# Answers in the banks of the scores with crossed heads, and a down product in a bank of its own in two halves

## The chip, the cores and the metric

The kernel runs on one core of one Trainium2 chip. The metric is the device time of one execution in microseconds (us). Five engines work in parallel, each through its own instruction stream and in order: PE (TensorE, matmuls and transposes), DVE (VectorE), ACT (ScalarE), POOL (GpSimd) and SP (SyncE, which issues most DMAs here). They are tied by semaphores. PE writes to PSUM, which has eight banks of 512 float32 columns by 128 partitions.

## What is computed

```python
# 4 batches, 8 heads, 768 steps, 48 channels a head
for t in range(S):                       # complex decay a, real input k v^T, real answer q S_re
    new_re = ar * S_re - ai * S_im
    new_im = ar * S_im + ai * S_re
    S_re, S_im = new_re + kv, new_im     # kv = k_t v_t^T per head, 48 x 48
    y[:, :, t] = einsum('bhd,bhde->bhe', q[:, :, t], S_re)
x = y laid out as (3072 tokens, 384)
x = max(x @ w1, x @ w2, x @ w3) @ w_out  # 384 -> 768 -> 384
# then a mixture of 8 experts: argmax routing, relu(x @ w1[e]) @ w2[e], gate
```

`a` is scaled to a magnitude of at most 0.999 first.

## The kernel before

The 3072 tokens are 24 chunks of 128. The program has two parts. The first is a loop over n = 0 to 25, which I call stages, written out by hand for each engine: the order of the calls in the source is the order on the engine. The second (from about 622 us) is the expert part, which the change does not touch.

Stage n works on three chunks at once:

- Chunk n, attention. `scores(n)` (PE, L1758) makes k·q for 8 heads into `sc` (two banks, 512 columns each). DVE's `mask(n)` (L1176) turns them into `att`. `keys_back(n)` (PE, L1768) transposes the keys into `tr`, ACT's `kp_copy` takes them out, `outer(n)` (PE, L1779) makes k v^T into the second bank of `yu`, DVE's `add_state` (L1201) adds it to the state, `rotation` (L1186 to L1191) decays the state. `answers(n)` (PE) has two pieces: `att` times v (L1791), and the old state times q (L1799), both into the first bank of `yu`. These last ones I call the state products. In chunks 0, 6, 12 and 18 a batch begins, and they are left out. ACT's `y_copy` (L739, L740) moves the answers to `y_end` and `x_raw`, SP moves small pieces between these two (`move_x`), ACT's `moe_x_hi` (L752) and DVE's `moe_x_lo` (L1152) split the result into two float32r parts.
- Chunk n-1, up products. `moe_up(t, g)` for g = 0 to 5 (PE, L1701, L1702, L1705: nine matmuls of 384 columns) goes to the two banks of `mm` in turn. ACT's `moe_copy` takes groups 0 and 3 into `h_sb`; DVE's `moe_max` (L1164) takes the maximum with groups 1, 2, 4 and 5.
- Chunk n-2, down product. `moe_ht` (PE, L1732) transposes `h_sb` into `tr` in halves, ACT's `moe_h_hi` (L763) and DVE's `moe_h_lo` (L1169) split it, `moe_down` (18 matmuls of 392 columns) writes to the second bank of `mm`, and ACT's `moe_out` (L769, L772, L774) reads it three times. `moe_up` group 1 of chunk n-1 needs the same bank, and waits on `x2_taken` for that.

A transposed `h_sb` half needs both of its maxima: `moe_ht(t, half)` waits on `p_maxed` for 4t + 2 half + 2.

Beside this runs the decay of `a`. Two chunks make a group (g = 0 to 11). Its 16 steps in a row are multiplied up by POOL (`chain_steps`, L2069 to L2073), its four blocks are joined by DVE (`join`, L1144 to L1148), ACT lays the result out (`stage_z`), and DVE makes decayed q and k for chunk n+1 from it (`z_norm` L1207, `z_newton`, `q_decay`, `k_decay`, up to L1233). The raw `a` is scaled ahead of that by ACT and DVE (`norm_square` to `norm_apply`, L1087 to L1117), stored to a scratch in device memory by SP, and loaded again in the layout of the chain (`load_ring`). So POOL's group g waits on a DMA which waits on DVE's `norm_apply` in an earlier stage. Tables (`norms_in`, `joins_early`, `joins_late`) say in which stage each of these steps stands; from group 6 on a group has one join late in stage 2g-3, one early and one late in stage 2g-2.

On PE a stage stands as: scores of two head pairs, transpose of the first half of chunk n-2, scores of the other pairs, up group 0, transpose of the second half, the whole down product, keys back, up group 1, outer, up group 2, answers, up groups 3 to 5.

Of the kernel before, what the change touches and what calls it, by code (L numbers as in the profile page):

```python
# [41 lines left out]
def attention_moe_program(nc, first_d, a_d, q_d, k_d, v_d, w_up, w_dn, emb, tau, e1, e2, q, k, v, a_re, a_im, an_d, x2_dram, out):  # L42
# [23 lines left out]
    with ctx:  # L66
# [595 lines left out]
        def _(act):  # L662
# [73 lines left out]
            def y_copy(n):  # L736
                act.wait_ge(y_done, n + 1)
                wait(act, xt_ready, n)
                nc.scalar.activation(y_end[:, :], yu[0:R, 0, KX * P:FREE], ACT.Copy).then_inc(y_copied, 1)  # L739
                nc.scalar.activation(x_raw[0:R, :, :], yu[0:R, 0, 0:KX * P].rearrange("p (k t) -> p k t", t=P), ACT.Copy).then_inc(y_copied, 1)  # L740

            def moe_copy(t, half):
                act.wait_ge(p_done, 6 * t + 3 * half + 1)
                if half == 0:
                    wait(act, ht_done, 2 * t)
# [20 lines left out]
            def moe_out(t, tile=None):  # L766
                at = ds(t if tile is None else tile, 1)
                act.wait_ge(x2_done, t + 1)
                nc.scalar.activation(z_all[:, at, :].rearrange("p t e -> p (t e)"), mm[:, 1, HD:NX], ACT.Copy) \  # L769
                    .then_inc(x2_taken, 1)  # L770
                wait(act, x2_stored, 16 * t)
                nc.scalar.activation(x2_sb[:, :], mm[:, 1, 0:HD], ACT.Copy).then_inc(x2_ready, 1)  # L772
                wait(act, x2_taken, 2 * t)
                nc.scalar.activation(mm[:, 1, 0:HD], mm[:, 1, 0:HD], ACT.Square,  # L774
# [78 lines left out]
            for n in range(NC + 2):  # L853
# [11 lines left out]
                if prev2:  # L865
                    moe_h_hi(n - 2, 0)
# [32 lines left out]
                if n == 0:  # L899
                    low_copy(range(14, 16))  # L900
                for m in norms:
                    norm_rsqrt(m, norm_of(m))
                for m in later[:1]:
                    norm_square(m, norm_of(m))
                if now:
                    y_copy(n)
                if n == 0:
                    low_copy(range(16, LOWS - KF + 3))
                if prev:
                    moe_copy(n - 1, 1)  # L910
# [3 lines left out]
            def steps(b):  # L914
                with act.Fori(0, CB) as part:
# [7 lines left out]
                    for x, (bank, dst) in enumerate(((sc, col_re), (tr, col_im), (sc, col_q), (tr, col_k))):  # L923
# [6 lines left out]
                    nc.scalar.activation(y_rows[:, :, :, 0:D], yu[:, 0, 0:KX * 2 * D].rearrange("p (k b d) -> p k b d", k=KX, b=2), ACT.Copy) \  # L930
                        .then_inc(y_copied, 1)
                    for x in range(KX):
                        ins = nc.scalar.activation(y_rows[:, x, :, D:HALF],
                                                   yu[:, 0, KX * 2 * D:HD].rearrange("p (b k r) -> p k b r", k=KX, b=2)[:, x, :, :], ACT.Copy)
# [1315 lines left out]
```

## Time and profile before

| | |
|---|---|
| time, median of 3 runs | 939.7 us (937.9 to 940.3) |
| the profiled execution | 938.67 us |
| its span in the profile | 936.9 us |
| PE busy | 836.2 us (89%) |
| DVE busy | 661.6 us (71%) |
| ACT busy | 441.9 us (47%) |
| POOL busy | 518.3 us (55%) |

A time line has the start and the length in us, the engine, the line, the output and inputs, the shape, the count, and in brackets the idle time just before with what ended it. "Mean ns" is that of one instruction. A float32 matmul (not float32r) is two rows in the profile. Busy shares are averages over stages with different limits, so the table does not name the bound of any one stage.

### The profile page before, as it was taken

The page shows a single profiled execution, that of the slowest core. Times are in us where ns is not written, and L with a number is a line of the kernel's source. Part 1 is how long each engine was busy: PE and PEld are TensorE (multiplying, and loading weights), DVE is VectorE, ACT ScalarE, POOL GpSimd, SP SyncE. Part 2 cuts the span into 40 slices and gives each one's busy share as a digit, 9 for nine tenths or more (in the row PEclk, how much of TensorE's full clock was granted, in tenths as well). Part 3 has the DMA queues.
Part 4 walks back from the last instruction along what each step waited for, and adds up shares of the span by engine and source line. Part 5 has one row for each costly group of instructions (what it writes and reads, how often), then busy time and mean ns, then how long its engine had stood idle before and what let it go on. Part 6 is the DMA issues. An engine that isn't in the chain of part 4 may idle for free.

```text
span 936.9 us, 18639 instructions
## 1 busy us (share of the span) xinstructions
PE 836.2 (89%) x6641; PEld 765.7 (82%) x6642; DVE 661.6 (71%) x1066; ACT 441.9 (47%) x817; POOL 518.3 (55%) x886
## 2 busy tenths in 40 slices
PE   0568899998998999999999999958999999999995
PEld 0445788887977898888898899857999999998894
DVE  5989789998897999999977755357533262647731
ACT  5686646574654566565443443231321142436611
POOL 1199989799999999998894000002332332324222
PEclk9769799999999999999999999985999999999998
DMA  9401142451424242432311110333711124236311
GB/s 304 117 20 31 65 112 83 100 163 56 130 63 101 73 124 80 110 84 64 90 41 41 51 56 20 107 121 128 280 59 34 42 64 165 94 126 225 129 35 43
DMA packets 41874, 89.72 MB, mean 96 GB/s; under 512 B 6264, under 2 KB 23680, under 8 KB 40480
## 3 DMA queue, kind: packets, MB, share of 16 engines
q1 hardware_dynamic: 37632, 76.04, 26.6%
q0 software_dynamic: 4160, 12.60, 4.0%
q8 instruction: 50, 0.82, 0.4%
q14 instruction: 32, 0.26, 0.1%
HBM read 69.74 MB, written 17.69 MB: 93 GB/s over the span
## 4 chain that ended last, share of the span: by engine, by line
PE 53%; POOL 17%; DVE 15%; issue 6%; ACT 5%; DMA 2%; SPq 1%; ACTq 0%; DVEq 0%; POOLq 0%
PE mm L1701 6%; PE mm L1705 5%; PE mm L1702 5%; POOL c_im L2070 4%; PE yu L1701 4%; POOL c_re L2069 4%; PE yu L1705 4%; PE yu L1702 4%; POOL ring L2073 4%; POOL ring L2072 3%; PE sc L1758 2%; PE tr L1970 2%; PE mm L1972 2%; PE tr L1972 2%; PE mm L1970 2%
## 5 line engine op out<-in xcount | busy, mean ns | idle before, releaser
L1701 PE MATMUL mm<-up_hi,x_hi 128*128 128x384 f32 x432 | 156.8, 363 | 23.0 <-ACT mm L774 9.7
L1702 PE MATMUL mm<-up_lo,x_hi 128*128 128x384 f32 x432 | 147.1, 341 | 0.0
L2069 POOL TENSOR_TENSOR c_re<-ring 112x128 f32<-112x128 f32 x165 | 104.3, 632 | 59.9 <-DVE ring L1117 36.2
L2070 POOL TENSOR_TENSOR c_im<-ring 112x128 f32<-112x128 f32 x165 | 118.8, 720 | 0.0
L2149 POOL DMA_INDIRECT out_rows<-g_o,rows_out x30 | 36.0, 1200 | 147.0 <-DVE g_o L1553 139.6
L1701 PEld LDWEIGHTS mm<-up_hi,x_hi 128*128 128x128 f32 x432 | 81.6, 189 | 38.8 <-ACT mm L774 14.7
L1705 PE MATMUL mm<-up_hi,x_lo 128*128 128x384 f32 x432 | 100.3, 341 | 3.0 <-DVE x_lo L1152 3.0
L2073 POOL TENSOR_TENSOR ring<-c_re,c_im 112x64 f32<-112x64 f32 x165 | 101.1, 613 | 0.0
L2125 POOL DMA_INDIRECT g_in<-x_scratch,rows_in x34 | 37.6, 1106 | 101.5 <-DVE rows_in L1516 76.1
L2072 POOL TENSOR_TENSOR ring<-c_re,c_im 112x64 f32<-112x64 f32 x165 | 83.9, 509 | 12.9
L1164 DVE TENSOR_TENSOR h_sb<-mm,h_sb 128x384 f32<-128x384 f32 x96 | 52.9, 552 | 46.7 <-PE mm L1705 44.9
L1705 PEld LDWEIGHTS mm<-up_hi,x_lo 128*128 128x128 f32 x432 | 78.8, 192 | 4.6 <-DVE x_lo L1152 4.6
L1701 PE MATMUL yu<-e_hi,gh_hi 128*128 128x384 f32 x240 | 82.4, 343 | 0.0
L1702 PEld LDWEIGHTS mm<-up_lo,x_hi 128*128 128x128 f32 x432 | 82.0, 190 | 0.0
L1702 PE MATMUL yu<-e_lo,gh_hi 128*128 128x384 f32 x240 | 80.9, 337 | 0.0
L1553 DVE TENSOR_SCALAR g_o<-yu,table_gate 128x384 f32 (+1 forms) x30 | 18.5, 617 | 70.3 <-POOLq L2145 36.1
L996 ACT ACTIVATE gh_hi<-tr 128x512 fp32r<-128x512 f32 x24 | 14.3, 598 | 102.5 <-PE tr L1972 98.0
L1418 DVE TENSOR_TENSOR e_lo<-raw,e_hi (+2 forms) x40 | 56.2, 1433 | 6.6 <-ACT e_hi L957 6.5
L1758 PE MATMUL sc<-q_t,k_t 48*128 48x128 f32 x768 | 57.7, 293 | 1.4 <-issue 1.2
L1758 PEld LDWEIGHTS sc<-q_t,k_t 48*128 48x128 f32 x768 | 48.9, 195 | 12.2 <-issue 12.2
L1701 PE MATMUL mm<-dn_hi,h_hi 128*128 128x392 f32 x144 | 51.9, 360 | 0.1
L1702 PE MATMUL mm<-dn_lo,h_hi 128*128 128x392 f32 x144 | 49.3, 343 | 0.0
(263 smaller groups left out, 2251.7 us busy)
## 6 DMA issues: line engine op xcount, KB each, us to landing
raw<-in_moe_w SPq DMA_DIRECT2D x16, 1536.0 KB, 9.0
a_dn<-in_a_laid SPq DMA_DIRECT2D x18, 384.0 KB, 7.0
an_scratch<-a_dn SPq DMA_DIRECT2D x18, 384.0 KB, 2.3
ring<-an_scratch SPq DMA_DIRECT2D x18, 384.0 KB, 5.8
q_in<-in_q_laid SPq DMA_DIRECT2D x24, 224.0 KB, 3.0
k_in<-in_k_laid SPq DMA_DIRECT2D x24, 224.0 KB, 3.1
v_in<-in_v_laid SPq DMA_DIRECT2D x24, 192.0 KB, 3.3
x_scratch<-x_sb SPq DMA_DIRECT2D x24, 192.0 KB, 2.6
```

The lines of the kernel that those rows point to most:

```text
L1164: nc.vector.tensor_tensor(hh, mm[:, (3 * half + w) % 2, 0:FH], hh, ALU.max).then_inc(p_maxed, 1)
L1418: nc.vector.tensor_tensor(flat(lo), flat(raw), flat(hi).bitcast(F32), ALU.subtract).then_inc(expert_lo, 1)
L1701: nc.tensor.matmul(out, hi[:, x, :], w_hi(x), start=(x == 0), stop=False)
L1702: nc.tensor.matmul(out, hi[:, x, :], w_lo(x), start=False, stop=False)
L1705: last = nc.tensor.matmul(out, lo[:, x, :], w_hi(x), start=False, stop=(x == K - 1))
L1758: last = nc.tensor.matmul(sc[:, b, h * P:(h + 1) * P], k_t[rows, x, h, :], q_t[n % 2][rows, x, h, :], start=(x == 0), stop=(x == 1))
L1970: nc.tensor.matmul(out, w_hi, x_hi[:, x, :], start=(x == 0), stop=False)
L2069: nc.gpsimd.tensor_tensor(c_re[:, 0:count, :, :], cur, bc(prev[:, :, 0, :], 2, 2), ALU.mult).then_inc(chain_prod, 1)
L2070: nc.gpsimd.tensor_tensor(c_im[:, 0:count, :, :], cur, bc(prev[:, :, 1, :], 2, 2), ALU.mult).then_inc(chain_prod, 1)
L2072: nc.gpsimd.tensor_tensor(cur[:, :, 0, :], c_re[:, 0:count, 0, :], c_im[:, 0:count, 1, :], ALU.subtract).then_inc(chain_step, 1)
L2073: nc.gpsimd.tensor_tensor(cur[:, :, 1, :], c_re[:, 0:count, 1, :], c_im[:, 0:count, 0, :], ALU.add).then_inc(chain_step, 1)
L2125: pool.indirect_dma_start(g_in[:, x, :], None, x2_dram, bass.IndirectOffsetOnAxis(ap=rows_in[x][:, :].bitcast(U32), axis=0)) \
```

## The change

It moves three things and reorders the stages around them.

1. The answers go to the two banks of `sc` (`answer_at`: columns 128, 512, 896 and 384 of the 1024) once the mask has read the scores. In head pairs 1 and 2 the two heads change sides (`side_of`): the head in partitions 0 to 47 of q and the state gives its answer to partitions 64 to 111. The weights w1 to w3 are laid out to match on the host. The state products are issued for two head pairs together, so that four in a row use the four combinations of row half and column half of the array. `scores(n+1)` now waits on `y_copied` for chunk n.
2. The down product goes to the first bank of `yu`, in two calls of nine matmuls. Group 1 of the up product no longer waits on `x2_taken` but on `p_maxed` (4t).
3. The first half of `h_sb` is transposed at the end of stage n-1 instead of in stage n, and split there.

```diff
             def moe_up(t, groups):
-                free = ((p_maxed, 4 * t - 1), (x2_taken, 2 * t), (p_copied, 2 * t + 1),
+                free = ((p_maxed, 4 * t - 1), (p_maxed, 4 * t), (p_copied, 2 * t + 1),
...
+            def moe_down(t, half):
+                out = yu[:, 0, 0:NX]
+                part = range(half * KX, (half + 1) * KX)
+                if half == 0:
+                    wait(pe, x2_taken, 2 * t)
+                pe.wait_ge(hh_ready, 2 * t + half + 1)
+                for x in part:
+                    nc.tensor.matmul(out, h_hi[:, x, :], dn_hi[:, x, :], start=(x == 0), stop=False)
+                    nc.tensor.matmul(out, h_hi[:, x, :], dn_lo[:, x, :], start=False, stop=False)
+                pe.wait_ge(ht_ready, 2 * t + half + 1)
+                for x in part:
+                    last = nc.tensor.matmul(out, h_lo[:, x, :], dn_hi[:, x, :], start=False, stop=(x == KF - 1))
...
+                    for both in ((0, 1), (3, 2)):
                         for x in range(2):
-                            for b in range(2):
-                                rows = rows_of(b)
-                                last = nc.tensor.matmul(yu[rows, 0, h * P:(h + 1) * P], st_t[rows, x, h, :], q_t[n % 2][rows, x, h, :],
-                                                        start=False, stop=(x == 1 and h == HP - 1))
+                            for h in both:
+                                for b in range(2):
+                                    rows = rows_of(b)
+                                    last = nc.tensor.matmul(answer[rows_of(side_of(h, b)), answer_at(h):answer_at(h) + P], st_t[rows, x, h, :],
+                                                            q_t[n % 2][rows, x, h, :], start=False, stop=(x == 1 and h >= 2))
...
 # PE's loop
                 if now:
-                    scores(n, range(0, HP // 2))
-                if prev2:
-                    moe_ht(n - 2, 0)
-                if now:
-                    scores(n, range(HP // 2, HP))
+                    scores(n)
...
+                if prev2:
+                    moe_down(n - 2, 0)
+                    moe_ht(n - 2, 1)
...
                     moe_up(n - 1, range(0, 1))
                 if prev2:
-                    moe_ht(n - 2, 1)
-                    moe_down(n - 2)
+                    moe_down(n - 2, 1)
...
-                if prev:
+                if prev and late_z:
                     moe_up(n - 1, range(2, 3))
                 if now:
                     answers(n)
+                if prev and not late_z:
+                    moe_up(n - 1, range(2, 3))
                 if prev:
-                    moe_up(n - 1, range(3, 6))
+                    moe_up(n - 1, range(3, 5))
+                    moe_ht(n - 1, 0)
+                    moe_up(n - 1, range(5, 6))
```

`late_z` is true in stages 1, 3 and 5 only. Three places show what stands in a row on an engine.

PE at the head of stage 15, from the scores to the second half's transpose and the down product. First as it stood, then as it stands; `tr<-ident,h_sb` is a transpose of `h_sb`, `dn_` the down weights, `up_` the up weights.

```order
L1758 MATMUL sc<-q_t,k_t 128x128 [waits masked,k_decayed,q_decayed]
L1758 MATMUL sc<-q_t,k_t 128x128 x7
L1732 MATMUL tr<-ident,h_sb 128x128 [waits p_maxed]
L1732 MATMUL tr<-ident,h_sb 128x128 x2
L1758 MATMUL sc<-q_t,k_t 128x128 x8
L1701 MATMUL mm<-up_hi,x_hi 128x384 [waits xh_ready,p_maxed]
```

```order
L1780 MATMUL sc<-q_t,k_t 128x128 [waits y_copied,k_decayed,q_decayed]
L1780 MATMUL sc<-q_t,k_t 128x128 x15
L1764 MATMUL yu<-dn_hi,h_hi 128x392 [waits hh_ready,x2_taken]
L1765 MATMUL yu<-dn_lo,h_hi 128x392
L1764 MATMUL yu<-dn_hi,h_hi 128x392
L1765 MATMUL yu<-dn_lo,h_hi 128x392
L1764 MATMUL yu<-dn_hi,h_hi 128x392
L1765 MATMUL yu<-dn_lo,h_hi 128x392
L1768 MATMUL yu<-dn_hi,h_lo 128x392 [waits ht_ready]
L1768 MATMUL yu<-dn_hi,h_lo 128x392 x2
L1754 MATMUL tr<-ident,h_sb 128x128 [waits p_maxed]
L1754 MATMUL tr<-ident,h_sb 128x128 x2
```

Group 0 comes next. Half of the down product now stands ahead of it, and so does the transpose of the second half, which waits for the last maximum of chunk n-2.

DVE at the head of stage 15, from the first split to the first maximum of the stage, before and after; `h_sb<-mm,h_sb` is a maximum, `a_dn` the scaled `a`, `att` the mask.

```order
L1164 TENSOR_TENSOR h_sb<-mm,h_sb 128x384 [waits p_maxed,p_copied,p_done] x2
L1152 TENSOR_TENSOR x_lo<-x_raw,x_hi 128x384 [waits xh_ready]
L1169 TENSOR_TENSOR h_lo<-tr,h_hi 128x384 [waits hh_ready]
L1114 SCALAR_TENSOR_TENSOR n_m<-n_la,n_rr 128x384 [waits rest_ready]
L1117 TENSOR_TENSOR a_dn<-a_dn,n_m 128x768 [waits scale_ready]
L1087 SCALAR_TENSOR_TENSOR n_m<-n_sq 128x384 [waits a_normed,asq_ready]
L1169 TENSOR_TENSOR h_lo<-tr,h_hi 128x384 [waits hh_ready]
L1176 TENSOR_TENSOR att<-sc,causal 128x512 [waits y_done,sc_done]
```

```order
L1181 TENSOR_TENSOR h_sb<-mm,h_sb 128x384 [waits p_maxed,p_copied,p_done]
L1186 TENSOR_TENSOR h_lo<-tr,h_hi 128x384 [waits hh_ready]
L1181 TENSOR_TENSOR h_sb<-mm,h_sb 128x384 [waits p_maxed,p_copied,p_done]
L1169 TENSOR_TENSOR x_lo<-x_raw,x_hi 128x384 [waits xh_ready]
L1131 SCALAR_TENSOR_TENSOR n_m<-n_la,n_rr 128x384 [waits rest_ready]
L1134 TENSOR_TENSOR a_dn<-a_dn,n_m 128x768 [waits scale_ready]
L1104 SCALAR_TENSOR_TENSOR n_m<-n_sq 128x384 [waits a_normed,asq_ready]
L1193 TENSOR_TENSOR att<-sc,causal 128x512 [waits y_done,sc_done]
L1193 TENSOR_TENSOR att<-sc,causal 128x512
L1186 TENSOR_TENSOR h_lo<-tr,h_hi 128x384 [waits hh_ready]
```

The first split of `h` has left the head of the stage, and the second has moved behind the two masks.

ACT in the middle of stage 15, from the scaling of `a` to the copy of group 3, before and after; `n_la`, `n_rr` and `n_sq` belong to the scaling of `a`.

```order
L685 ACTIVATE n_la<-n_m 128x384 [waits sum_ready]
L687 ACTIVATE n_la<-n_la 128x384 [waits sumln_ready]
L690 ACTIVATE n_rr<-n_la 128x384 [waits scale_ready,r0_ready]
L674 ACTIVATE n_sq<-a_dn 128x768 [waits m2_ready,a_loaded3]
L739 ACTIVATE y_end<-yu 112x128 [waits xt_ready,y_done]
L740 ACTIVATE x_raw<-yu 112x384
L746 ACTIVATE h_sb<-mm 128x384 [waits p_done]
```

```order
L749 ACTIVATE y_end<-sc 112x128 [waits xt_ready,y_done]
L750 ACTIVATE x_raw<-sc 112x384
L695 ACTIVATE n_la<-n_m 128x384 [waits sum_ready]
L697 ACTIVATE n_la<-n_la 128x384 [waits sumln_ready]
L700 ACTIVATE n_rr<-n_la 128x384 [waits scale_ready,r0_ready]
L684 ACTIVATE n_sq<-a_dn 128x768 [waits m2_ready,a_loaded3]
L756 ACTIVATE h_sb<-mm 128x384 [waits ht_done,p_done]
L773 ACTIVATE h_hi<-tr 128x384 [waits x2_done,ht_done]
```

The copy of the answers has moved ahead of the scaling of `a`, and the split of the first half of `h` has come in behind the copy of group 3. In the same way `kp_copy` has moved ahead of `moe_out`. On DVE the first maximum of the up product has moved ahead of the early joins in even stages. The rows of SP and POOL are the same.

## Rows read from the trace of the kernel before

**Rows 1.** Busy time by stage: stages 10, 14, 17, 18 and 20.
```profile
core 0: us, PE busy (x) PEld busy (x) DVE busy (x) ACT busy (x) POOL busy (x), PEclk, DMA share, GB/s
...
295.95:321.78 25.83, 22.85 (x199) 20.91 (x198) 24.11 (x37) 13.04 (x26) 24.25 (x40) 0.93 0.22 67
...
386.63:408.24 21.61, 21.24 (x199) 19.41 (x198) 21.20 (x34) 13.06 (x26) 20.28 (x34) 1.00 0.18 61
...
451.71:473.92 22.21, 21.29 (x199) 19.41 (x198) 19.51 (x31) 9.60 (x20) 18.52 (x36) 1.00 0.37 96
473.92:493.65 19.73, 19.36 (x167) 17.71 (x166) 14.69 (x22) 9.29 (x19) 18.40 (x36) 1.00 0.15 47
...
515.27:536.88 21.61, 21.24 (x199) 19.41 (x198) 15.86 (x28) 9.18 (x19) 1.22 (x6) 1.00 0.13 42
```

**Rows 2.** PE's time line in stage 15, from the down product to group 3.
```profile
412.83 0.49 PE L1732 MATMUL tr<-ident,h_sb 128*128 128x128 f32 x3
413.08 0.42 PE L1701 MATMUL mm<-dn_hi,h_hi 128*128 128x392 f32 x1
...
416.37 0.93 PE L1768 MATMUL tr<-ident,k_t 112*128 112x112 f32 x8
417.67 0.44 PE L1701 MATMUL mm<-up_hi,x_hi 128*128 128x384 f32 x1 [0.37 <-ACT mm L774]
...
419.45 1.13 PE L1779 MATMUL yu<-v_in,kp 128*64 128x48 f32 x32
420.51 0.44 PE L1701 MATMUL mm<-up_hi,x_hi 128*128 128x384 f32 x1
...
422.28 1.09 PE L1791 MATMUL yu<-att,v_in 128*64 128x128 f32 x16
423.30 1.95 PE L1799 MATMUL yu<-q_t,st_t 48*48 48x128 f32 x32
425.18 0.45 PE L1701 MATMUL mm<-up_hi,x_hi 128*128 128x384 f32 x1
```

**Rows 3.** DVE's time line, from the split of stage 14 to that of stage 16.
```profile
388.53 0.73 DVE L1152 TENSOR_TENSOR x_lo<-x_raw,x_hi 128x384 fp32r<-128x384 f32 x1
...
411.07 0.73 DVE L1152 TENSOR_TENSOR x_lo<-x_raw,x_hi 128x384 fp32r<-128x384 f32 x1
411.72 0.55 DVE L1169 TENSOR_TENSOR h_lo<-tr,h_hi 128x384 fp32r<-128x384 f32 x1
412.19 0.54 DVE L1114 SCALAR_TENSOR_TENSOR n_m<-n_la,n_rr 128x384 f32<-128x384 f32 x1
...
414.62 1.27 DVE L1176 TENSOR_TENSOR att<-sc,causal 128x512 f32<-128x512 f32 x2
415.81 0.54 DVE L1186 TENSOR_TENSOR st_same<-st_x,rot 112x384 f32<-112x384 f32 x1
...
419.56 0.56 DVE L1164 TENSOR_TENSOR h_sb<-mm,h_sb 128x384 f32<-128x384 f32 x1 [1.16 <-PE mm L1705]
...
420.64 0.56 DVE L1201 TENSOR_TENSOR st_x<-yu,st_t 112x384 f32<-112x384 f32 x1 [0.52 <-PE yu L1779]
...
423.04 0.55 DVE L1164 TENSOR_TENSOR h_sb<-mm,h_sb 128x384 f32<-128x384 f32 x1
...
432.25 0.72 DVE L1152 TENSOR_TENSOR x_lo<-x_raw,x_hi 128x384 fp32r<-128x384 f32 x1
```

**Rows 4.** POOL's time line: the first steps of groups 4 and 7.
```profile
172.26 0.46 POOL L2069 TENSOR_TENSOR c_re<-ring 112x128 f32<-112x128 f32 x1 [4.71 <-DMA ring<-an_scratch]
...
296.54 0.87 POOL L2069 TENSOR_TENSOR c_re<-ring 112x128 f32<-112x128 f32 x1 [0.17 <-POOL ring L2073]
```

**Rows 5.** DVE's time line: the first join of group 6, in stage 9.
```profile
296.41 0.69 DVE L1144 TENSOR_TENSOR l_re<-ring 112x512 f32<-112x512 f32 x1 [3.49 <-POOL ring L2073]
```

**Rows 6.** PE's time line: idle at 301, 604 and 610 us.
```profile
301.29 0.42 PE L1701 MATMUL mm<-up_hi,x_hi 128*128 128x384 f32 x1 [2.61 <-DVE h_sb L1164]
...
604.05 0.41 PE L1701 MATMUL mm<-up_hi,x_hi 128*128 128x384 f32 x1 [1.67 <-ACT x_hi L752]
...
610.55 0.44 PE L1701 MATMUL mm<-up_hi,x_hi 128*128 128x384 f32 x1 [1.14 <-ACT mm L774]
```

**Rows 7.** Busy time in a short stretch after PE's wait at 301 us.
```profile
302.00:304.00 2.00, 2.00 (x8) 1.97 (x7) 1.97 (x4) 1.67 (x3) 1.92 (x4) 0.50 0.00 0
```

More of the change, by code:

```diff
@@ L522, in low_block, with answer_at, side_of @@
             return raw, hi, lo, bank
+        answer = sc[:, :, :].rearrange("p b f -> p (b f)")
+        def answer_at(h):
+            return P * (1 + 3 * h) if h < KX else 3 * P
+        def side_of(h, b):
+            return 1 - b if h in (1, 2) else b
         def rows_of(h):
@@ L1310, in _ @@
                     norm_m2(m, norm_of(m))
+                if now and not late_z:
+                    mask(n)
                 if prev2:
@@ L1315, in _ @@
                         join(g, number)
-                if now:
+                if now and late_z:
                     mask(n)
@@ L1323, in _ @@
                     norm_m2(m, norm_of(m))
-                for g, number in early if n not in (1, 3, 5) else ():
+                if more and n >= 2 and not late_z:
+                    z_norm(n + 1)
+                if prev:
+                    moe_max(n - 1, 0, 1)
+                for g, number in early if not late_z else ():
                     join(g, number)
-                if more:
+                if more and (n < 2 or late_z):
                     z_norm(n + 1)
@@ L1733, in moe_ht, with scores @@
                 last.then_inc(ht_done, 1)
[L1735 to L1754 removed]
+            def moe_down(t, half):
[10 more added lines that the diff above has]
+                    last = nc.tensor.matmul(out, h_lo[:, x, :], dn_hi[:, x, :], start=False, stop=(x == KF - 1))
+                if half == 1:
+                    last.then_inc(x2_done, 1)
+            def scores(n):
+                pe.wait_ge(q_decayed, n + 1)
+                pe.wait_ge(k_decayed, n + 1)
+                wait(pe, y_copied, 2 * n)
+                for h in range(HP):
                     for x in range(2):
@@ L1827, in _ @@
                     pe.wait_ge(lo_copied, LOWS - KF)
+                if prev2:
+                    if n == 2:
+                        pe.wait_ge(lo_copied, LOWS)
+                    moe_down(n - 2, 0)
+                    moe_ht(n - 2, 1)
+                if n == NC:
+                    pe.wait_ge(y_copied, 2 * NC)
+                    pe.wait_ge(low_step, 4)
+                    nc.tensor.matmul(sc[0:1, 0, 0:2], low_col[0:R, 1:2], ones[0:R, 0:2], start=True, stop=True).then_inc(low_step, 1)
                 if prev:
```

93 lines of the change are left out of this document (38 added, 55 removed).

## The prediction, made before the changed kernel was run

> **What bounds the kernel now.** I read the busy time by stage first, to see which engine has no slack where. In stage 20 PE is busy for 21.24 of 21.61 us and DVE for 15.86: PE sets the pace [rows 1]. In stage 14 PE has 21.24 and DVE 21.20 of 21.61; in stage 10 DVE has 24.11 of 25.83, PE 22.85 and POOL 24.25 [rows 1]. So the last stages belong to PE, those around 14 to PE and DVE together, the early ones to DVE and POOL. The chain of waits is no help here, since it changes engine several times in a stage; the time lines tell more. PE's shows what a stage is made of [rows 2]. DVE's shows how long a stage takes when DVE is late: from split to split 411.07 - 388.53 = 22.54 us in stage 14, with no wait in it, and 432.25 - 411.07 = 21.18 us in stage 15, with waits of 1.16 and 0.52 [rows 3]. Even stages from 6 on have early joins, odd ones don't, so DVE falls behind in even stages and catches up in odd ones. Together that is 43.7 us a pair, a little more than PE's 2 x 21.61. POOL runs groups 4 to 6 without a gap: 296.54 - 172.26 = 124.3 us, 41.4 a group, and in stage 9 DVE waits 3.49 us for the end of group 6 [rows 4, 5].
>
> **State products in four quarters.** 32 rows take 425.18 - 423.30 = 1.88 us, 59 ns each [rows 2]; two halves of the array work side by side. Four quarters are not in this trace. The lower bound is the rate at which PE passes small matmuls: the outer products, 32 rows of 48 columns, take 420.51 - 419.45 = 1.06 us, 33 ns each [rows 2]. The upper bound, if the crossed pairs queue behind each other, is twice the time of now, 3.8 us. I take 1.06, because two row halves and two column halves each overlap already (the products with `att`, 16 rows in 1.02 us, use two column halves) and nothing in the rows sets the combination apart. That saves 0.82 us a stage, where PE is the bound. The other price, 1.88, is a rival below. The products with `att` keep their shape of 128 columns; only padding columns leave, so nothing.
>
> **The down product's bank.** The wait of 0.37 us on the last read of `mm` goes [rows 2]; it stands in each stage from 2 on. The two halves have the same 18 matmuls. The reads by ACT are the same three, on another bank, whose next writer comes almost a stage later. Nothing.
>
> **A stage of PE, then.** 21.61 - 0.82 - 0.37 = 20.4 us; a stage without state products, 19.73 - 0.37 = 19.4 [rows 1, 2].
>
> **The scores wait on the copy of the answers.** Behind the answers PE now has groups 2 to 5 (three groups in stages 1, 3, 5), at 422.28 - 420.51 = 1.77 us each [rows 2], 5.3 to 7 us. The copy is two instructions on ACT and has moved ahead of the scaling of `a` there. If the cover were gone, the scores and all of PE behind them would wait. Nothing here. The copy of group 3 now comes behind that scaling, but group 5, which waits for it, has three groups and a transpose ahead. The opposite order in even stages, maximum before early joins, costs DVE only what it waits for PE, next.
>
> **Where DVE is late: stages 10 to 16.** Count from the moment at which DVE has the last maximum of chunk n-2, with PE standing at the transpose of the second half. PE: transpose 0.25, group 0 1.7, the six high matmuls of the second half 6/18 of 3.29 = 1.1, so it wants `h_lo` at 3.05 [rows 2]. DVE: from split to mask 3.55, less 0.47 for the `h_lo` that has left the head (412.19 - 411.72), so 3.1; less another 0.47, since the second `h_lo` now stands behind the masks; masks 1.19, then `h_lo` 0.47: 4.3 [rows 3]. So PE waits 1.2 us in the middle of the down product, which it did not before. Then low part 0.55, keys back 0.93, group 1 1.78: done at 7.6; outer 1.06: 8.6; answers 2.08: 10.7; group 2 1.77: 12.5 [rows 2]. DVE comes to the first maximum 7.33 us after the split (419.56 - 1.16 - 411.07), less 0.47 = 6.9, and waits until 7.6. It adds the state at 8.7. It comes to the second maximum 423.04 - 420.64 = 2.4 later, 11.1, and in an odd stage waits until 12.5, because group 2 has moved behind the answers. From there 9.2 us to the next split and 0.47 for the moved `h_lo`: 22.2 us in place of 21.18 [rows 3]. An even stage has an early join behind the first maximum, which covers the two later waits, so only the first remains: 22.54 + 0.7 = 23.2. So the change costs 1.0 in stages 11, 13 and 15 and 0.7 in 14 and 16, and about nothing in 10 and 12, where a wait for `h_hi` or for the outer product goes in return: together +4.5 us. What PE saves there is lost in waits for DVE.
>
> **Before stage 10.** The pace is that of POOL. Its group 4 starts after a DMA wait of 4.71 us [rows 4], which ends with DVE's scaling in stage 4; DVE reaches it earlier by one `h_lo` (0.5) and by what stages 1 to 3 save. I work with 3 us, between 1.5 and the 4.7 at which POOL itself is the limit. Through groups without a gap this comes down to the join of group 6 [rows 5], so stage 10 begins 3 us earlier.
>
> **From stage 17 on** PE sets the pace again: 22.21 - 20.4 = 1.8 in stage 17, 0.4 in stage 18, 1.2 in each of 19 to 23: -8.2 us [rows 1].
>
> **The end.** Stage 24 has PE waits of 1.67 and 1.14 us [rows 6]. The first is hidden by half a down product, the second is on the bank that is no longer shared; the second half of the last down product then waits about 0.5 for its split. -2.5 us.
>
> **Sum:** -3 + 4.5 - 8.2 - 2.5 = -9.2 us on the profiled execution's 938.67, 929.5; the median of the runs is 1.0 above it, so 930.5 us.
>
> **Rivals.**
> 1. DVE's waits don't appear, since PE is not quite as early as I count, or DVE's order is shifted by them only once. Then stages 10 to 16 lose nothing, or up to 1 us of seven stages is gained: 926 to 919. For it: DVE's nets contain contention with POOL that I can't separate. Against it: both orders are fixed, and the sums above use start times of one stage.
> 2. The state products don't overlap in quarters. PE's stage is 21.2: 0.82 x 6 stages = 4.9 lost at the end, and group 2 later by 0.82 in stages 11, 13, 15, 2.5: 938. In the rows, the two heads of a pair have different row halves and the same bank (`rows_of` and `yu` in the old `answers`), and run at 59 ns a row [rows 2], the pace of the products with `att` (64 ns), which use all rows and two column halves. So two row halves in one bank cost nothing that shows. The Trainium skill (TensorEngine Tiling (Array Packing), Gotcha 1: PSUM Pressure) says that different row tiles cannot access the same PSUM bank simultaneously. By it the crossed pairs, which put both row halves in each bank, gain nothing, and the answer is this rival's time; but by it the products of now would not overlap either, and the trace disagrees with that.
> 3. Slower: PE's clock falls. After the wait of 2.61 us at 301 [rows 6] the granted clock was 0.50 (the 1.2 GHz level) from 302 to 304 [rows 7], and PE had kept full clock while it worked without a gap. In stages 10 to 16 PE will now stand still for 2 to 3 us in a stage, in two or three pieces. If each of the seven stages has one fall, group 1 and 2 come some 1.5 us later (8 matmuls in 2 us [rows 7] where 11 fit), and DVE with them: +10.5, so 941. It decides as soon as one piece of the idle time is as long as that of 301; the pieces that I count are 1.2 and under 2.
> 4. The crossed products queue: 3.8 us. +2.7 in some ten stages, 957 or more.
>
> **Chances.** Forecast 0.45 (own range 925 to 936), rival 1 0.24, rival 2 0.14, rival 3 0.14, rival 4 0.03. A difference under 0.3% (936.9 to 942.5) is about what a measurement of this kernel can't tell from none. Faster by more: 0.45 x 0.95 + 0.24 + 0.14 x 0.3 = 0.71. Same: 0.02 + 0.10 + 0.05 = 0.17. Slower: the rest of rival 3 and rival 4, 0.12. The range that leaves out 0.2 is 919 to 942.
>
> **What would show it.** Right: the state products' 32 rows in 1.1 us; stage 20 in 20.4 us; no wait of PE on the third read of the down product; a PE wait on `h_lo` in stages 11 to 16, and a DVE wait of over 1 us on group 2 in 11, 13 and 15; DVE's stage 15 at 22.2 us; POOL's group 4 at about 169. Wrong: state products at 1.9; stage 20 at 21 or more; stages 11 to 16 shorter than before; a granted clock of 0.50 in them; PE waiting for `y_copied` at the scores.

## The result and the profile of the changed kernel

The changed kernel takes 923.3 us (median of 4 runs, 921.7 to 924.3), the kernel before 938.8 beside it. The ratio is 0.983, with a 95% interval of 0.981 to 0.985: 1.7% faster, where 0.9% was forecast (930.5 us, range 919 to 942). The profiled execution has a span of 922.5 us in place of 936.9. So 14.4 us are gone, of which the forecast had 9.2. The median lies in the stated range, but outside the 925 to 936 that the forecast gave as its own, and among the times of rival 1.

First the busy time by stage, with the columns of [rows 1]: stages 10, 15 and 21, then two short stretches for the clock.

```profile
293.87:319.19 25.32, 21.31 (x199) 19.80 (x199) 21.86 (x35) 13.01 (x26) 23.66 (x41) 0.93 0.22 75
...
408.07:430.12 22.05, 20.26 (x199) 18.22 (x198) 19.56 (x32) 12.86 (x26) 19.10 (x35) 1.00 0.39 96
532.82:552.27 19.45, 19.45 (x199) 18.36 (x199) 13.48 (x24) 9.42 (x19) 1.62 (x6) 1.00 0.15 42
302.00:304.00 2.00, 2.00 (x9) 1.90 (x9) 1.97 (x4) 2.00 (x5) 1.92 (x3) 0.50 0.00 0
120.00:124.00 4.00, 4.00 (x35) 3.56 (x34) 0.60 (x2) 2.72 (x8) 3.61 (x11) 0.53 0.98 155
```

Stage 21 takes 19.45 us, with PE busy from end to end, and stages 20 and 22 take the same; before, stage 20 took 21.61 [rows 1], and so did 21 and 22. Stage 15 has PE busy for only 20.26 of 22.05 us. So the last stages are shorter by more than forecast, and those around 15 are no longer PE's at all.

PE's time line in stage 15 of the changed kernel, from the down product's first half to group 2, answers to [rows 2].

```profile
412.65 0.81 PE L1768 MATMUL yu<-dn_hi,h_lo 128*128 128x392 f32 x3 [1.25 <-DVE h_lo L1186]
...
417.22 0.81 PE L1768 MATMUL yu<-dn_hi,h_lo 128*128 128x392 f32 x3 [0.54 <-DVE h_lo L1186]
417.86 0.93 PE L1789 MATMUL tr<-ident,k_t 112*128 112x112 f32 x8
418.56 0.42 PE L1723 MATMUL mm<-up_hi,x_hi 128*128 128x384 f32 x1
...
422.25 1.09 PE L1819 MATMUL sc<-q_t,st_t 48*48 48x128 f32 x32
423.28 0.44 PE L1723 MATMUL mm<-up_hi,x_hi 128*128 128x384 f32 x1
```

The 32 rows of the state products take 423.28 - 422.25 = 1.03 us, 32 ns each, in place of 1.88. From the keys' transposes to group 1 it is 418.56 - 417.86 = 0.70 us in place of 417.67 - 416.37 = 1.30 [rows 2], and nothing is waited for there. New are the two waits on `h_lo` (L1768 is the low part of the down product), 1.25 us in the first half and 0.54 in the second. A view that adds up what PE waits for (us in all, times, longest) has 23 of them in the whole kernel; each of stages 11 to 17 has two:

```profile
PE yu L1768 <- DVE h_lo L1186: 25.4, 23, 4.0
```

DVE's time line from the split of stage 15 to the next answers to [rows 3].

```profile
412.98 0.54 DVE L1169 TENSOR_TENSOR x_lo<-x_raw,x_hi 128x384 fp32r<-128x384 f32 x1
...
415.42 1.27 DVE L1193 TENSOR_TENSOR att<-sc,causal 128x512 f32<-128x512 f32 x2
416.62 0.54 DVE L1186 TENSOR_TENSOR h_lo<-tr,h_hi 128x384 fp32r<-128x384 f32 x1
...
420.42 0.56 DVE L1181 TENSOR_TENSOR h_sb<-mm,h_sb 128x384 f32<-128x384 f32 x1 [0.55 <-PE mm L1727]
...
421.50 0.56 DVE L1218 TENSOR_TENSOR st_x<-yu,st_t 112x384 f32<-112x384 f32 x1 [0.52 <-PE yu L1800]
...
425.17 0.56 DVE L1181 TENSOR_TENSOR h_sb<-mm,h_sb 128x384 f32<-128x384 f32 x1 [1.18 <-PE mm L1727]
...
434.36 0.63 DVE L1169 TENSOR_TENSOR x_lo<-x_raw,x_hi 128x384 fp32r<-128x384 f32 x1
```

The second `h_lo` comes behind the masks, at 416.62, and PE's second wait ends with it. DVE then waits 0.55 for group 1, 0.52 for the outer product and 1.18 for group 2, which now stands behind the answers. The cycle is 434.36 - 412.98 = 21.38 us, against 21.18 in [rows 3].

POOL and PE's idle time, for [rows 4] and [rows 6]: the first steps of POOL's groups 4 and 7, then PE at 301 and 607 us.

```profile
172.41 0.74 POOL L2094 TENSOR_TENSOR c_re<-ring 112x128 f32<-112x128 f32 x1 [4.25 <-DMA ring<-an_scratch]
...
296.68 0.87 POOL L2094 TENSOR_TENSOR c_re<-ring 112x128 f32<-112x128 f32 x1 [0.17 <-POOL ring L2098]
```

```profile
301.21 1.33 PE L1768 MATMUL yu<-dn_hi,h_lo 128*128 128x392 f32 x3 [4.01 <-DVE h_lo L1186]
...
607.38 0.45 PE L1764 MATMUL yu<-dn_hi,h_hi 128*128 128x392 f32 x1 [0.58 <-ACT h_hi L773]
```

Groups 4 to 6 still run without a gap, 124.3 us, and in this execution group 4 starts where it did before. The wait of 1.67 us at the end is gone, and so is the one of 1.14 [rows 6].

### The profile page after: what moved, and what is told of

It reads as the page before. It is cut to its first block, busy times and chain, and to the rows that moved or that the text cites. A ratio compares the mean times of both kernels' runs of the same rounds, so it can differ in the third digit from the quotient of the medians.

```text
span 922.5 us, 18638 instructions
## 1 busy us (share of the span) xinstructions
PE 809.4 (88%) x6641; PEld 745.6 (81%) x6642; DVE 658.0 (71%) x1066; ACT 442.1 (48%) x817; POOL 519.9 (56%) x886
## 4 chain that ended last, share of the span: by engine, by line
PE 50%; DVE 19%; POOL 17%; issue 8%; ACT 3%; DMA 2%; ACTq 0%; DVEq 0%; SPq 0%; POOLq 0%
POOL c_im L2095 5%; PE yu L1723 4%; POOL c_re L2094 4%; PE yu L1727 4%; PE yu L1724 4%; POOL ring L2098 4%; PE mm L1723 4%; PE mm L1727 3%; POOL ring L2097 3%; PE mm L1724 3%; PE yu L1768 2%; PE tr L1995 2%; PE mm L1995 2%; PE mm L1997 2%; PE tr L1996 2%
## 5 line engine op out<-in xcount | busy, mean ns | idle before, releaser
L2095 POOL TENSOR_TENSOR c_im<-ring 112x128 f32<-112x128 f32 x165 | 123.3, 747 | 0.0
L2098 POOL TENSOR_TENSOR ring<-c_re,c_im 112x64 f32<-112x64 f32 x165 | 96.4, 584 | 0.0
L2097 POOL TENSOR_TENSOR ring<-c_re,c_im 112x64 f32<-112x64 f32 x165 | 83.8, 508 | 12.9
L1013 ACT ACTIVATE gh_hi<-tr 128x512 fp32r<-128x512 f32 x24 | 14.4, 600 | 102.1 <-PE tr L1997 100.6
L1768 PE MATMUL yu<-dn_hi,h_lo 128*128 128x392 f32 x144 | 37.3, 368 | 25.4 <-DVE h_lo L1186 25.4
L1764 PE MATMUL yu<-dn_hi,h_hi 128*128 128x392 f32 x144 | 52.6, 366 | 0.6 <-ACT h_hi L773 0.6
L1768 PEld LDWEIGHTS yu<-dn_hi,h_lo 128*128 128x128 f32 x144 | 25.0, 193 | 33.4 <-DVE h_lo L1186 33.4
L1780 PEld LDWEIGHTS sc<-q_t,k_t 48*128 48x128 f32 x768 | 45.6, 190 | 6.7 <-issue 6.7
```

The costliest lines, as they stand in the source:

```text
L1764: nc.tensor.matmul(out, h_hi[:, x, :], dn_hi[:, x, :], start=(x == 0), stop=False)
L1768: last = nc.tensor.matmul(out, h_lo[:, x, :], dn_hi[:, x, :], start=False, stop=(x == KF - 1))
L1780: last = nc.tensor.matmul(sc[:, b, h * P:(h + 1) * P], k_t[rows, x, h, :], q_t[n % 2][rows, x, h, :], start=(x == 0), stop=(x == 1))
L2095: nc.gpsimd.tensor_tensor(c_im[:, 0:count, :, :], cur, bc(prev[:, :, 1, :], 2, 2), ALU.mult).then_inc(chain_prod, 1)
L2097: nc.gpsimd.tensor_tensor(cur[:, :, 0, :], c_re[:, 0:count, 0, :], c_im[:, 0:count, 1, :], ALU.subtract).then_inc(chain_step, 1)
L2098: nc.gpsimd.tensor_tensor(cur[:, :, 1, :], c_re[:, 0:count, 1, :], c_im[:, 0:count, 0, :], ALU.add).then_inc(chain_step, 1)
```

## Where the 14.4 us come from

I take DVE's splits `x_lo` as marks where DVE sets the pace and PE's stage starts where PE does. DVE's splits of stages 10 and 17, before and after:

```profile
301.18 0.73 DVE L1152 TENSOR_TENSOR x_lo<-x_raw,x_hi 128x384 fp32r<-128x384 f32 x1
...
454.88 0.73 DVE L1152 TENSOR_TENSOR x_lo<-x_raw,x_hi 128x384 fp32r<-128x384 f32 x1
```

```profile
301.54 0.54 DVE L1169 TENSOR_TENSOR x_lo<-x_raw,x_hi 128x384 fp32r<-128x384 f32 x1
...
457.35 0.54 DVE L1169 TENSOR_TENSOR x_lo<-x_raw,x_hi 128x384 fp32r<-128x384 f32 x1
```

| stretch | forecast | measured |
|---|---|---|
| up to the split of stage 10 | -3 | +0.4 |
| from there to the split of stage 17 | +4.5 | +2.1 |
| from there to PE's stage 18 (473.92, now 474.28) | -1.8 | -2.1 |
| stages 18 to 23 (24 begins at 601.7, now 591.1) | -6.4 | -11.0 |
| stage 24, up to the routing (626.25, now 612.36) | -2.5 | -3.2 |
| behind it | 0 | -0.5 |
| sum | -9.2 | -14.4 |

The terms before stage 10 and for stages 18 to 23 are off by over 3 us, in opposite directions, and the one for stages 10 to 16 (the second row) by 2.4. The experiments look at each.

## Experiments

Times are medians; each is compared with runs of the kernel before on the same chip (938 to 939 us). "Changed" stands for the changed kernel.

**Heads not crossed.** In no pair do the two heads change sides, so the state products use two of the four quarters of the array. The banks and the rest are as changed.

```
-            return 1 - b if h in (1, 2) else b
+            return b
...
-        heads[:, 1:3] = heads[:, 1:3, ::-1].copy()
```

> The changed kernel without crossed heads (the up weights laid out to match), all else kept: the state products then use two quarters of the array. If the overlap of four quarters is what shortened them, their 32 rows go back from 1.02 us to about 1.9 us, stages 20 to 22 from 19.45 to 20.3 us, and the kernel to 929 to 932 us. If the shorter stages come from the new places (banks, neighbours) and not from the quarters, the rows stay near 1.0 us and the time at 923 us.

Measured: 929.7 us (928.5 to 932.3), ratio 0.991, interval 0.988 to 0.994. Stage 20 and the first row of its state products:

```profile
515.04:535.33 20.29, 20.29 (x199) 19.20 (x198) 15.62 (x29) 9.30 (x19) 0.00 (x0) 1.00 0.16 47
```

```profile
526.61 1.95 PE L1819 MATMUL sc<-q_t,st_t 48*48 48x128 f32 x32
```

A stage of PE is 20.29 us, 0.84 more than with crossing, and the rows are back at 1.88 (the next group starts at 528.49). So the crossing is worth its 0.82 us a stage where PE sets the pace, 6.4 us in all. In stage 15 DVE waits 2.18 us for group 2 in place of 1.18.

**The old wait alone.** The down product keeps its own bank, but group 1 waits for the residual sum's read of it, and ACT does that read ahead of `kp_copy`, as before.

```
                     wait(pe, *free[g])
+                    if g == 1:
+                        wait(pe, x2_taken, 2 * t)
```

> The down product stays in its own bank, but group 1 waits again on the third read of it, and ACT reads it ahead of the keys as before: the old wait alone. The forecast priced it at its idle time, 0.37 us a stage: stages 20 to 22 at 19.8 us, the kernel at 925.5 us. What the two traces suggest (keys back to group 1 took 1.30 us before and takes 0.70 now): 0.6 us a stage, 20.05 us, and 927 us.

Measured: 934.4 us (932.0 to 937.5), ratio 0.995, interval 0.994 to 0.997. PE in stage 21:

```profile
546.09 0.93 PE L1791 MATMUL tr<-ident,k_t 112*128 112x112 f32 x8
547.48 0.42 PE L1723 MATMUL mm<-up_hi,x_hi 128*128 128x384 f32 x1 [0.46 <-ACT yu L784]
```

The idle time shown is 0.46 us, but from the transposes to group 1 it is 547.48 - 546.09 = 1.39 us against 0.70 without the wait. The price of the wait is the 0.69, and that is also what the stage grows by (20.13 to 20.14). In the whole kernel it costs 11.1 us, more than the 2 to 4 that were expected. It delays group 1 also where DVE waits for it: DVE's wait for group 1 in stage 15 is 1.20 us in place of 0.55, and from the split of stage 10 to that of 17 it is 4.7 us more.

**Order alone.** Both of these together: what stays of the change is the order of the instructions (but for ACT's read, which stands as before) and the place of the results.

> The changed kernel without both of its measures: heads not crossed (state products at 59 ns a row, as in the experiment without crossing), and the wait of group 1 on the residual sum that is read on ACT from the down product's bank, as in the experiment with the old wait. What stays is the order: down product in two halves, scores in one block behind the answers' copy. Theory (the two measures add up, and the order is worth what is left): stages 20 to 22 at 19.45 + 0.85 + 0.69 = 21.0 us, 0.6 under the kernel before; in all 6.4 + 11.1 us more than the changed kernel, 941, so the order alone gains nothing or loses 2 us, because stages 10 to 16 pay for its waits on h_lo and group 2. Rival (the measures overlap, the order has a gain of its own): 933 to 937.

Measured: 943.8 us (942.3 to 946.2), ratio 1.005, interval 1.003 to 1.007. Its stage 20, and DVE's splits of stages 15 and 16:

```profile
526.97:547.95 20.98, 20.52 (x200) 19.25 (x199) 15.63 (x29) 9.29 (x19) 0.00 (x0) 1.00 0.16 46
```

```profile
420.43 0.55 DVE L1169 TENSOR_TENSOR x_lo<-x_raw,x_hi 128x384 fp32r<-128x384 f32 x1
...
443.68 0.62 DVE L1169 TENSOR_TENSOR x_lo<-x_raw,x_hi 128x384 fp32r<-128x384 f32 x1
```

Stages of PE are 20.98 us, 0.6 shorter than before, as expected. But DVE's stage 15 takes 23.25 us in place of 21.18, with waits of 1.18 for group 1, 0.52 for the outer product and 2.16 for group 2, and from the split of stage 10 to that of 17 it is 163.2 us in place of 153.7. The new order is slower on its own; my count of what it costs DVE was right in kind. The two measures pay for that and bring the gain: 943.8 - 923.3 = 20.5 us. One alone brings 14.0 (bank, from 943.8 to 929.7) or 9.4 (crossing, from 943.8 to 934.4).

**The second `h_lo` ahead of the masks.** On DVE, in all stages but 3 and 5, the split comes before the masks.

```
+                if prev2:
+                    moe_h_lo(n - 2, 1)
                 if now and not late_z:
                     mask(n)
-                if prev2:
-                    moe_h_lo(n - 2, 1)
```

> One swap on DVE: the split of the second half of h stands ahead of the two masks again. Theory (the 25.4 us of PE waits on this split hold up group 1, and through it DVE): the waits fall under 8 us, stages 10 to 17 are 0.5 to 1 us shorter each, the kernel takes 917 to 920 us. Rival (in those stages DVE's own work, or the later group 2, is the bound): the waits of PE fall, those of DVE on group 2 grow, and the kernel stays at 922 to 924 us.

Measured: 917.4 us (915.7 to 918.2), ratio 0.977, interval 0.974 to 0.980. DVE from the split of stage 15 to that of stage 16:

```profile
407.67 0.54 DVE L1169 TENSOR_TENSOR x_lo<-x_raw,x_hi 128x384 fp32r<-128x384 f32 x1
...
410.60 0.54 DVE L1186 TENSOR_TENSOR h_lo<-tr,h_hi 128x384 fp32r<-128x384 f32 x1
...
419.13 0.56 DVE L1181 TENSOR_TENSOR h_sb<-mm,h_sb 128x384 f32<-128x384 f32 x1 [1.14 <-PE mm L1727]
...
428.64 0.63 DVE L1169 TENSOR_TENSOR x_lo<-x_raw,x_hi 128x384 fp32r<-128x384 f32 x1
```

The cycle is 20.97 us in place of 21.38, and stage 14's 22.30 in place of 22.64. Only the wait of 1.14 us for group 2 is left; those for group 1 and the outer product are gone, since PE had been held up by that `h_lo`. Stages 20 to 22 are unchanged (19.41 to 19.42). PE's waits on that split are 18.7 us in all in place of 25.4, where under 8 were expected; most of what is left is in front of the first half (1.24 us in stage 15). So the place of one instruction of 0.47 us costs the changed kernel 5.9 us.

**Group 2 ahead of the answers in odd stages.** It gives DVE the second maximum earlier; even stages stay.

```
-                if prev and late_z:
+                early_up = n % 2 == 1
+                if prev and early_up:
                     moe_up(n - 1, range(2, 3))
```

> The changed kernel with group 2 of the up product ahead of the answers again in all odd stages (in stages 1, 3 and 5 it is so already). Theory (in late odd stages DVE waits 1.2 us for group 2 because it stands behind the answers): that wait goes, the odd stages 9 to 15 are up to 1 us shorter, 919 to 921 us. Rival (PE stands between two waits for DVE's split there, so the time only moves to another wait): 922.5 to 924 us. In stages 19 and 21 one more change of shape between outer products and answers should cost 0.1 us each.

Measured: 919.9 us (919.0 to 922.3), ratio 0.980, interval 0.977 to 0.982. The wait for group 2 is gone, and odd stages of DVE take 20.69, 20.21 and 20.69 us (stages 11, 13, 15), even ones 22.81 and 22.65 (14 and 16; changed: 22.64 and 22.99). It is the term "until 12.5, because group 2 has moved behind the answers" of the prediction, by itself 3.4 us; the interval overlaps that of the changed kernel, but the stages differ clearly. In stage 21, where PE sets the pace, the group that now stands between the outer products and the answers makes the stage 19.78 us in place of 19.45, though the matmuls are the same.

**Both of them.**

> Both the swap on DVE (second split of h ahead of the masks, 917.4 us by itself) and group 2 ahead of the answers in odd stages. If the remaining DVE wait on group 2 (1.1 to 1.2 us in odd stages) is on the path: 914 to 916 us, with stage 15 from split to split at 19.8 us. If not: 917 to 918 us.

Measured: 916.2 us (915.7 to 917.0), ratio 0.976, interval 0.974 to 0.978. Together they bring 7.1 us, less than the sum of the two (5.9 + 3.4), and hardly more than the first alone. Stage 15 takes 20.28 us, where 19.8 were expected. A third engine is next, DVE at the late join of stage 15:

```profile
420.93 0.69 DVE L1161 TENSOR_TENSOR l_re<-ring 112x512 f32<-112x512 f32 x1 [1.03 <-POOL ring L2099]
```

DVE now waits 1.03 us there for POOL's groups, and 1.04 in stage 17. That this makes up the whole difference isn't shown.

**Groups 1 and 2 ahead of the down product's second half and the outer product**, from stage 2 on, with the second `h_lo` ahead of the masks.

```
+                early_up = n >= 2
+                if prev and early_up:
+                    moe_up(n - 1, range(1, 2))
                 if prev2:
                     moe_down(n - 2, 1)
...
+                if prev and early_up:
+                    moe_up(n - 1, range(2, 3))
                 if now:
                     outer(n)
```

> The swap on DVE, and on PE groups 1 and 2 of the up product ahead of the second half of the down product and of the outer products (stages 2 on). Both maxima then never wait in late stages, but the state's sum waits for a later outer product, about 1.2 us by my count. If what DVE waits for in sum decides: 916 to 918 us, no better than the swap alone; if PE's waits on the split decide (18.7 us left in the swap alone): 913 to 915 us. The keys' copy and the outer products have one group between them, so PE should not wait there.

Measured: 913.5 us (913.2 to 916.1), ratio 0.973, interval 0.971 to 0.976: the fastest of all, 25 us under the kernel before. DVE at the join of group 6 shows what bounds it next:

```profile
292.45 0.69 DVE L1161 TENSOR_TENSOR l_re<-ring 112x512 f32<-112x512 f32 x1 [6.10 <-POOL ring L2103]
```

Stage 9 now ends with a wait of 6.10 us for POOL, and PE waits 7.12 for the `h_lo` behind it (at 297.10). What stages 1 to 9 gain beyond POOL's pace is lost there.

**A transpose inside the scores.** From stage 18 on the second half's transpose stands between the scores' halves, to see what a change of the matmul's form costs.

```
                 if now:
-                    scores(n)
+                    scores(n, range(0, HP // 2))
+                if prev2 and n > 17:
+                    moe_ht(n - 2, 1)
+                if now:
+                    scores(n, range(HP // 2, HP))
```

> From stage 18 on the transpose of the second half of h stands between the scores of two head pairs, as the first half's did before; nothing else. Theory (a stage on PE lost about 1 us beyond the forecast because tiles of other shapes no longer stand in between): stages 20 to 22 go from 19.45 to 19.8 us or more, and the kernel to 925 us. Rival (the shape changes cost nothing, the gain is elsewhere): 19.45 us and 923 us.

Measured: 935.5 us (933.2 to 936.3), ratio 0.996, interval 0.994 to 0.998. PE in stage 21:

```profile
540.27 0.55 PE L1754 MATMUL tr<-ident,h_sb 128*128 128x128 f32 x3 [1.07 <-DVE h_sb L1181]
```

That doesn't answer the question: the transpose there waits for DVE's last maximum (1.07 us here, 2.13 and 2.19 in stages 18 and 19), and the price of the form can't be told from that of the wait. It shows why the new order has that transpose behind a half of the down product.

**Two matmuls inside the scores.** The same question with work that waits for nobody: from stage 18 on, the first two matmuls of the down product stand between the halves.

```
+                if now and n > 17:
+                    scores(n, range(0, HP // 2))
+                    moe_down_start(n - 2)
+                    scores(n, range(HP // 2, HP))
```

> The changed kernel, but from stage 18 on the first two matmuls of the down product stand between the two halves of the scores. Nothing is added, and nobody waits for them. Theory (a change of the matmul's shape costs PE time of its own, which the old order had once more, inside the scores): 2 x some 0.1 us more in each of six stages, stages 20 to 22 at 19.6 to 19.7 us in place of 19.45, the kernel 0.6 to 1.5 us longer than the changed one. Rival (the scores are only faster for another reason, e.g. a wait behind the first half): 19.45, no difference.

Measured: 924.4 us (923.2 to 924.8), ratio 0.985, interval 0.982 to 0.987; the intervals of this and the changed kernel overlap, but the stages differ clearly. PE in stage 20:

```profile
511.18 1.16 PE L1787 MATMUL sc<-q_t,k_t 48*128 48x128 f32 x16
512.27 0.44 PE L1760 MATMUL yu<-dn_hi,h_hi 128*128 128x392 f32 x1
...
512.82 1.16 PE L1787 MATMUL sc<-q_t,k_t 48*128 48x128 f32 x16
513.91 0.44 PE L1770 MATMUL yu<-dn_hi,h_hi 128*128 128x392 f32 x1
```

Stages 20 to 22 take 19.84 to 19.85 us, 0.40 more than the changed kernel's 19.45, for the same matmuls. The 32 score rows take 2 x 1.09 us in place of 1.98, and the pair 0.55 in place of two times 0.18. So each change from one form to the other costs about 0.2 us, and a return trip 0.4, twice what I had expected. Form stands here for all in which the two sorts of matmul differ (rows used, columns, output bank); the parts were not taken apart.

**Both kernels again, unaltered**, for a second profiled execution.

> The changed kernel once more, unaltered, for a second profiled execution of its head. Theory (the head differs from execution to execution, since waits and clock falls in stages 1 to 3 are a matter of tenths of a microsecond): POOL's group 4 starts anywhere from 167 to 173, 172.41 was one draw. Rival (the changed order itself keeps it at 172): 172 to 173 again.

> The kernel before once more, unaltered, for a second profiled execution. Theory of the varying head: group 4 of POOL starts within 167 to 173, not at 172.26 again; stages 20 to 22 again at 21.6 us and x_lo from stage 10 to 17 again about 153.7 us apart. Rival: 172.3 within 0.5.

Measured: 921.9 us and 938.8 us, one run each. POOL's group 4, DVE's splits of stages 10 and 17, and a short stretch of the changed kernel's second execution:

```profile
168.18 0.47 POOL L2094 TENSOR_TENSOR c_re<-ring 112x128 f32<-112x128 f32 x1 [2.01 <-DMA ring<-an_scratch]
```

```profile
298.15 0.54 DVE L1169 TENSOR_TENSOR x_lo<-x_raw,x_hi 128x384 fp32r<-128x384 f32 x1
...
454.92 0.54 DVE L1169 TENSOR_TENSOR x_lo<-x_raw,x_hi 128x384 fp32r<-128x384 f32 x1
```

```profile
120.00:124.00 4.00, 4.00 (x79) 3.63 (x75) 2.80 (x5) 2.14 (x6) 3.77 (x7) 1.00 0.98 226
```

The last line is its busy time and clock from 120 to 124 us, where the first execution has 0.53.

Group 4 starts at 168.18 us in place of 172.41, and DVE's split of stage 10 comes at 298.15, 3.0 us ahead of before. In the experiment with two matmuls inside the scores, whose code is the same up to stage 17, it is 170.90 and 299.29, and in the one with a transpose inside the scores, of which the same holds, 171.01 and 299.58. The kernel before repeats itself: 172.42 and 300.96, against 172.26 and 301.18. So the changed kernel's head varies by 4 us from execution to execution, the old one's two are alike.

## Why the forecast was right, and where its steps were not

**State products: right.** 1.03 us in place of 1.88, forecast 1.06. The crossed pairs put both row halves of the array into each bank, and a row takes 32 ns. Rivals 2 and 4 are out, and the experiment without crossing shows that the saving is due to the crossing. The Trainium skill (TensorEngine Tiling (Array Packing), Gotcha 1: PSUM Pressure) has row tiles not use one bank at a time; by it, as the prediction reads it, the rows would have stayed at 59 ns. The trace disagrees, for row halves that write different partitions of the bank. A variant in which all four quarters at once write to one bank, so that both row halves meet on the same partitions, was planned (1.9 us or more and 929 us if that can't be, 1.0 us and 923 us if the bank doesn't matter), but it never ran; what happens there is open.

**The bank wait: right in kind, too small.** I took its idle time, 0.37 us [rows 2]. The wait costs 0.60 to 0.69 in a stage, 0.23 more than the view shows as idle; the experiment with the old wait shows it. The rows say where the 0.23 is: the row of the keys' transposes ends 0.93 us after its start, and idle time is counted from there, but where nothing is waited for group 1 starts 0.70 after it. The Trainium skill (TensorE: Matmul & The Clock Gate, Single matmul latency) has a single bf16 matmul pay a fixed part of some 0.17 us at full clock, the drain among it; the 0.23 here is of that order, though what makes it up wasn't measured.

**A stage of PE: the term that was mis-sized.** Forecast 20.4 us, measured 19.45. The head of stage 20 before, and of stage 21 now, with the first half's transposes near that stage's end:

```profile
515.27 1.16 PE L1758 MATMUL sc<-q_t,k_t 48*128 48x128 f32 x16
516.36 0.55 PE L1732 MATMUL tr<-ident,h_sb 128*128 128x128 f32 x3
516.84 1.16 PE L1758 MATMUL sc<-q_t,k_t 48*128 48x128 f32 x16
517.93 0.44 PE L1701 MATMUL mm<-up_hi,x_hi 128*128 128x384 f32 x1
```

```profile
532.82 2.06 PE L1780 MATMUL sc<-q_t,k_t 48*128 48x128 f32 x32
534.81 0.44 PE L1764 MATMUL yu<-dn_hi,h_hi 128*128 128x392 f32 x1
...
550.27 0.49 PE L1754 MATMUL tr<-ident,h_sb 128*128 128x128 f32 x3
550.52 0.42 PE L1723 MATMUL mm<-up_hi,x_hi 128*128 128x384 f32 x1
```

Of the 2.16 saved, 0.85 are the state products, 0.60 the wait, 0.20 the scores in one block (1.98 in place of 2.18), 0.23 the first half's transposes, which take 0.25 between two groups in place of 0.48 between two halves of the scores. Some 0.28 are spread over the other borders. I had costed the reordering on PE at nothing, because it has the same matmuls; but their borders are not free. The experiment with two matmuls inside the scores shows such a price by itself, 0.40 us for one more return trip, about what the scores and transposes give back here. The experiments give the same 2.16 in another way: the order alone saves 0.63 in such a stage (21.61 to 20.98), the crossing 0.84 and the bank 0.69. The forecast had these at 0, 0.82 and 0.37. In each of stages 20 to 23 the wait's 0.23 and the borders' 0.7 are nearly all that the forecast missed, some 3.7 of the 4.6 us in this term.

**The wait on `h_lo` and DVE's loss: right, smaller.** The waits are where the count put them: in stage 15 DVE's are 0.55, 0.52 and 1.18 us, forecast 0.7, 0.5 and 1.4. PE's own wait for the second `h_lo` is 0.54, forecast 1.2: PE comes there later, because it has first stood 1.25 us for the first `h_lo`, ahead of the first half's low part, which the count left out. The rest of DVE's cycle is 19.1 us where the count had 19.6 from start times of one stage. Part of that is that the split `x_lo` itself is done in 0.54 us where it took 0.73 [rows 3]; why is open, since another instruction stands behind it and POOL runs at another phase. Where POOL has almost no work, from stage 20 on, that split takes 0.54 to 0.56 in both kernels, so its overlap with POOL is a likely cause, not a tested one. Stage 15 is so 21.4 us in place of 22.2, and stages 10 to 16 lose 2.1 us in the first execution, 3.1 in the second (156.8 us between the splits), where I had 4.5. The order alone loses 9.5 there; the measures give 7.4 of it back. Rival 1, that the waits don't appear, is out, though the time lies in its range: the gain is PE's at the end.

**Before stage 10: true in three executions of four, not in the one profiled first.** +0.4 us in the first execution, -3.0 in the second, -1.9 and -1.6 in the two experiments that have the same code up to stage 17; the prediction had -3, with bounds of 1.5 and 4.7. The step from group 4 through POOL's groups to DVE's join held both times. What the two differ in is the clock. In stage 2 PE waits 2.88 us for `h_lo` in the first, 2.84 in the second, a wait that the change has added. Behind it the granted clock is 0.53 from 120 to 124 us in the first (above) and 1.00 in the second, where PE passes 79 matmuls there in place of 35 (shapes differ). DVE then waits 3.09 us for group 1 in the first and 0.51 in the second, and from its split of stage 2 to that of stage 3 it takes 26.36 and 23.64 us. In the two experiments, with 2.84 and 2.86 us of the same wait, the clock is 0.79 on the mean from 116 to 124. So the gain can be 3 us, and a fall of the clock can cost all of it; which happens isn't settled by the length of the wait. Added up in steps of 2 us from 80 to 310, PE is at the lower level for 24 us in the first execution, 14 in the second, 14 and 18 in the two experiments, and 14 in both executions of the kernel before. The spans of the two are 922.5 and 920.1 us.

**Rival 3, the clock:** it came in part, but ahead of the stages for which it was written. In the first execution the clock reaches 0.50 to 0.52 in stages 1, 2, 3, 5, 6 and 10. After the wait of 4.01 us at 301 the clock is 0.50, the 1.2 GHz level, from 302 to 304, as it was before after 2.61 us [rows 6, 7], and stage 10 has 0.93 on the mean as before [rows 1]. In stages 11 to 16, with pieces of 0.5 to 1.4 us, it stays at 1.00. The point at which the rival was to decide, a piece as long as that of 301, was not reached there. Nor is the length of one piece a safe sign. The first row is of the kernel before, behind a wait of 1.94 us that ended at 105.53, the second of the changed kernel, behind one of 2.40 us that ended at 267.65:

```profile
108.00:110.00 2.00, 2.00 (x19) 1.78 (x16) 1.05 (x3) 0.61 (x1) 1.84 (x7) 0.50 0.05 12
268.00:270.00 2.00, 2.00 (x14) 1.97 (x13) 1.96 (x3) 0.45 (x2) 1.92 (x3) 1.00 0.00 0
```

**The end:** -3.2 against -2.5, with 0.58 us left of the wait that I had put at 0.5.

The errors were +3.4 before stage 10, -2.4 in 10 to 16, -4.6 in 18 to 23, and some -1.6 elsewhere. That they partly cancel is luck: with the head of the second execution, where that term came out as forecast, the gain is 16.8 us, not 14.4, against 9.2. Both prices that failed were read off the view: the stall at the idle time that it shows, and the borders at nothing, because it shows none.

## What to carry to other kernels

A stall of PE costs more than its idle time: compare the distance between the two neighbours with the same distance where nobody waits. A new order with the same work has a price of its own, on PE at each change of form, and on the other engines wherever a short instruction now stands in front of what PE wants (one of 0.47 us cost 5.9 here). So try an order and the measures that come with it apart: here the order alone was 0.5% slower than the old kernel.

## What the runs showed of the hardware

- Four quarters of the array at once take rows of 48 x 128 at 32 ns, with two row halves in the same bank (1.03 us for 32 rows); two quarters take 59 ns.
- An exposed wait of PE with 0.37 to 0.46 us idle costs 0.60 to 0.69.
- A change between score rows and matmuls of 392 columns costs about 0.2 us, at full clock, both ways.
- PE's granted clock was 0.50 behind single waits of 1.94, 2.61 and 4.01 us, and 1.00 behind one of 2.40 us and through pieces of up to 1.4 us, two in a stage. After a wait of 2.9 us in stage 2 it fell in one execution (0.53) and not in another (1.00, after 2.84).
- A row of matmuls ends in the view 0.23 us after the point at which the next could start (0.93 against 0.70 us for the keys' eight transposes).
